# Attention with weight splitting: loads reordered, four weight chunks per slot, one threshold comparison moved to VectorE

## What is computed

```python
scores = scale * q @ k.T
kth = the 32nd largest of each row
scores = where(scores >= kth, scores, -1e9)
attn = exp(scores - max) / (sum + 1e-9)
x = (attn @ v), heads side by side           # 2304 x 512
out = ((x @ w_a) * (x @ w_b)) @ w_out
```

## Time and profile before

| | us |
|---|---|
| median of 3 runs | 920.54 (920.47 to 922.51) |
| the profiled execution | 920.49 |
| its span in the trace | 918.6 |
| TensorE matmul busy | 832.0 (91%) |
| VectorE busy | 725.4 (79%) |
| ScalarE busy | 593.5 (65%) |
| GpSimd busy | 736.1 (80%) |

### The profile page before, as it was taken

The page is one execution under the profiler, slowest core; times in us unless marked ns, Lnnn a source line. Parts: engine busy times, 40 slices in busy tenths (PEclk is TensorE's granted clock), DMA queues, the critical chain, the costliest instruction groups (busy, mean ns, idle before and its releaser), DMA issues.

```text
span 918.6 us, 17902 instructions
## 1 busy us (share of the span) xinstructions
PE 832.0 (91%) x6368; PEld 682.5 (74%) x6368; DVE 725.4 (79%) x1595; ACT 593.5 (65%) x1296; POOL 736.1 (80%) x618
## 2 busy tenths in 40 slices
PE   2357668999999999999999999999999999999998
PEld 1134446887788888877888888877888888888897
DVE  2778889997798999977999898888988999995000
ACT  3466667666677776666766776666677777775322
POOL 3699998987788889877888888877888888889232
PEclk9999999999999999999999999999999999999999
DMA  6422431112331121122321211123222111211221
GB/s 167 127 72 75 143 111 52 41 43 67 80 90 41 53 59 47 44 66 73 96 54 41 65 41 42 48 60 102 67 55 64 50 47 42 61 35 47 70 60 56
DMA packets 83175, 60.92 MB, mean 66 GB/s; under 512 B 60816, under 2 KB 60816, under 8 KB 83088
## 3 DMA queue, kind: packets, MB, share of 16 engines
q1 hardware_dynamic: 83088, 59.79, 23.5%
HBM read 51.90 MB, written 7.86 MB: 65 GB/s over the span
## 4 chain that ended last, share of the span: by engine, by line
PE 71%; POOL 12%; ACT 7%; issue 5%; DVE 2%; DMA 1%; SPq 1%; ACTq 0%; POOLq 0%
PE ps L428 31%; PE ps L441 14%; PE ps L396 7%; PE ps L373 7%; PE ps L363 6%; POOL keep L641 5%; POOL scores L649 4%; POOL w_lo L628 2%; ACT scores L528 2%; PE ps L359 1%; ACT scores L521 1%; ACT probs_t L545 1%; PE ps L388 1%; ACT scores L536 1%; DMA stage<-in_w 1%
## 5 line engine op out<-in xcount | busy, mean ns | idle before, releaser
L641 POOL TENSOR_SCALAR keep<-scores,best 128x576 f32<-128x576 f32 x144 | 319.1, 2216 | 11.2 <-POOL scores L649 5.9
L707 DVE MAX8 best<-work 128x8 f32<-128x576 f32 x432 | 304.6, 746 | 0.0
L428 PE MATMUL ps<-x_hi,w_hi 128*128 128x256 f32 x864 | 262.9, 304 | 3.1 <-ACT x_lo L555 3.1
L428 PE MATMUL ps<-x_hi,w_lo 128*128 128x256 f32 x864 | 243.3, 282 | 0.0
L428 PE MATMUL ps<-x_lo,w_hi 128*128 128x256 f32 x864 | 243.0, 281 | 0.0
L717 DVE MATCH_REPLACE8 work<-best,work 128x576 f32<-128x576 f32 x288 | 211.6, 742 | 0.0
L649 POOL TENSOR_TENSOR scores<-scores,keep 128x576 f32<-128x576 f32 x144 | 204.4, 1419 | 3.5
L428 PEld LDWEIGHTS ps<-x_hi,w_hi 128*128 128x128 f32 x864 | 162.5, 188 | 35.4 <-issue 26.9
L428 PEld LDWEIGHTS ps<-x_lo,w_hi 128*128 128x128 f32 x864 | 163.1, 189 | 0.9
L428 PEld LDWEIGHTS ps<-x_hi,w_lo 128*128 128x128 f32 x864 | 162.6, 188 | 0.0
L655 POOL TENSOR_TENSOR ab<-ab 128x256 f32<-128x256 f32 x108 | 79.4, 735 | 84.3 <-ACT ab L561 84.3
(11 more groups left out here) (50 smaller groups left out, 1050.8 us busy)
## 6 DMA issues: line engine op xcount, KB each, us to landing
wo_lo<-x_scratch SPq DMA_DIRECT2D x108, 256.0 KB, 2.7
stage<-in_w SPq DMA_DIRECT2D x36, 256.0 KB, 2.8
q_rows<-in_q SPq DMA_DIRECT2D x72, 64.0 KB, 2.6
k_rows<-in_k SPq DMA_DIRECT2D x32, 128.0 KB, 2.4
v_rows<-in_v SPq DMA_DIRECT2D x32, 128.0 KB, 2.5
out<-stage SPq DMA_DIRECT2D x15, 256.0 KB, 2.6
x_scratch<-wo_lo SPq DMA_DIRECT2D x12, 256.0 KB, 2.0
out<-stage SPq DMA_DIRECT2D x6, 128.0 KB, 2.4
```

Source lines behind the costliest of these rows:

```text
L428: last = mm(ps_ab[:, which, :], w[:, c, o:o + P], x[:, g % 2, kb, :], start=(kb == 0 and i == 0), stop=(kb == KB - 1 and i == 2))
L641: V.tensor_scalar(keep[:], scores[:, u % ROWS, j, 0:S], best[:, u % 2, j, TOPK - 1:TOPK], NEG, ALU.is_lt, ALU.mult).then_inc(keep_ready, 1)
L707: ins = V.max(best[:, s % 2, j, 8 * r:8 * r + 8], src)
```

## The change

Three things are done, for the slots up to 8 only.

- Loads: SyncE starts with K of both first pairs, then Q of unit 1, then four weight chunks; each pair of V is loaded in a slot of its own, -2 to 1. Q of unit 0 is issued by ScalarE, ahead of its first instruction.
- Weights: four chunks in each of slots 0 to 8 and none before slot 0, with four `stage` buffers instead of three. So `between(s, 0)` now holds a chunk too.
- Comparison: for units 0 to 7, VectorE compares tile 0 (L733 of the changed kernel) behind the search of its unit, into `work`, tile 0, which that search no longer needs; GpSimd adds it to the scores right behind `shifts`, ahead of the slot's first cut. VectorE's first replacement in tile 0 of the next unit, which writes `work`, waits for that mask (`mask_done`). Tile 1 stays on GpSimd.

```diff
--- before.py
+++ after.py
@@ -34,7 +34,6 @@
     WB0 = KB * DFF // WC
     WO0 = 2 * WB0
     ROWS = 4
-    STAGES = 3
     RING = 4
     QBUF = 3
 
@@ -71,7 +70,7 @@
                 at += 1
             PREP_AT[at] = (b, p)
     PREPS = [PREP_AT[at] for at in sorted(PREP_AT)]
-    V_AT = {}
+    V_AT = {p - 2: [(0, p)] for p in range(KB)}
     for b in range(1, BATCHES):
         for p in range(KB):
             V_AT.setdefault(last_unit(b - 1, p) + 3, []).append((b, p))
@@ -97,12 +96,10 @@
     def o_step(F):
         return 3 * (F + 2) + 2
 
-    W_COUNT = {-2: 3, -1: 4, 0: 5, 1: 3, 2: 3, 3: 3, 4: 3, 5: 3, 6: 3, 7: 3, 8: 3}
-    W_AT, w_next = {}, 0
-    for s in sorted(W_COUNT):
-        W_AT[s] = list(range(w_next, w_next + W_COUNT[s]))
-        w_next += W_COUNT[s]
-    assert w_next == WCH
+
+    W_EACH = 4
+    STAGES = 4
+    W_AT = {s: list(range(s * W_EACH, (s + 1) * W_EACH)) for s in range(WCH // W_EACH)}
 
     def w_of(s, n, parts):
         mine = W_AT.get(s, [])
@@ -123,6 +120,7 @@
         w_lo = sb("w_lo", [P, WO0, WC], fp32r)
         wo_lo = sb("wo_lo", [P, RING, WC], fp32r)
         stage = sb("stage", [P, STAGES, WC])
+        y = stage
         ident = sb("ident", [P, P])
         neg_ident = sb("neg_ident", [P, P], fp32r)
         k_rows = sb("k_rows", [P, NB, P])
@@ -145,7 +143,6 @@
         ab = sb("ab", [P, 2, 2, G])
         h_hi = sb("h_hi", [P, 2, G], fp32r)
         h_lo = sb("h_lo", [P, 2, G], fp32r)
-        y = stage
 
         ps = ctx.enter_context(nc.psum_tensor("ps", [P, 8, 512], fp32))
         ps_s = ps[:, 0:2, 0:HALF]
@@ -176,6 +173,7 @@
         chain = sem("chain")
         kth_ready = sem("kth_ready")
         keep_ready = sem("keep_ready")
+        early_ready = sem("early_ready")
         mask_done = sem("mask_done")
         e_ready = sem("e_ready")
         inv_ready = sem("inv_ready")
@@ -204,10 +202,15 @@
         def is_tail(u):
             return UNITS[u][1] == FULL
 
+
+        def compared_early(u, j):
+            return j == 0 and u + 1 in W_AT
+
         def preps_before(u):
             b, t, pairs, place = UNITS[u]
             return max(PREPS.index((b, p)) for p in pairs) + 1
 
+        EARLY = [u for u in range(NU) if compared_early(u, 0)]
         PIECES = []
         for g in range(GROUPS):
             pieces = []
@@ -240,7 +243,7 @@
                              ).then_inc(ld_k, 16)
 
             def load_q(u):
-                if not unit(u):
+                if not unit(u) or u == 0:
                     return
                 b, t, pairs, place = UNITS[u]
                 wait(sp, qt_done, u - QBUF + 1)
@@ -297,13 +300,10 @@
                         store_y(F // NF)
 
             load_k(0)
-            load_q(0)
+            load_k(1)
+            load_q(1)
             for c in range(STAGES):
                 load_w(c)
-            load_q(1)
-            load_k(1)
-            for p in range(KB):
-                load_v(0, p)
             for s in range(FIRST, LAST):
                 for b, p in V_AT.get(s, []):
                     load_v(b, p)
@@ -589,6 +589,8 @@
                 for c in w_of(s, part, 4):
                     split_hi(c)
 
+            act.dma_start(q_rows[:, 0, 0:2 * D].rearrange("p (h d) -> p h d", h=2),
+                          q[0:2, 0:P, :].rearrange("h p d -> p h d")).then_inc(ld_q[0], 16)
             act.wait_ge(s_ident, 2)
             A.mul(neg_ident[:], ident[:], -1.0).then_inc(s_negid, 1)
             copy_k(0)
@@ -626,7 +628,6 @@
                     wait(pool, st_wo[n % RING], 16 * (n // RING))
                     to = wo_lo[:, n % RING, :]
                 V.tensor_tensor(to, stage[:, c % STAGES, :], w_hi[:, c, :], ALU.subtract).then_inc(w_lo_done, 1)
-
             def shifts(u):
                 if not unit(u):
                     return
@@ -634,7 +635,7 @@
                 V.tensor_scalar(neg_max[:, u % 2, :], best[:, u % 2, :, 0], -SCALE, None, ALU.mult)
 
             def below(u, j):
-                if not unit(u):
+                if not unit(u) or compared_early(u, j):
                     return
                 pool.wait_ge(kth_ready, 2 * u + j + 1)
                 wait(pool, mask_done, 2 * u + j)
@@ -645,7 +646,11 @@
                 if not unit(u):
                     return
                 row = scores[:, u % ROWS, j, 0:S]
-                pool.wait_ge(keep_ready, 2 * u + j + 1)
+                if compared_early(u, j):
+                    pool.wait_ge(early_ready, EARLY.index(u) + 1)
+                    V.tensor_tensor(row, row, work[:, j, :], ALU.add).then_inc(mask_done, 1)
+                    return
+                pool.wait_ge(keep_ready, sum(not compared_early(n // 2, n % 2) for n in range(2 * u + j + 1)))
                 V.tensor_tensor(row, row, keep[:], ALU.add).then_inc(mask_done, 1)
 
             def after_step(n):
@@ -672,9 +677,12 @@
                             pattern=[[-1, P]], channel_multiplier=1).then_inc(s_ident, 1)
             for s in range(FIRST, LAST):
                 shifts(s - 1)
+                if unit(s - 1) and compared_early(s - 1, 0):
+                    masked(s - 1, 0)
                 below(s - 1, 0)
                 between(s, 0)
-                masked(s - 1, 0)
+                if unit(s - 1) and not compared_early(s - 1, 0):
+                    masked(s - 1, 0)
                 between(s, 1)
                 below(s - 1, 1)
                 between(s, 2)
@@ -714,10 +722,16 @@
                         for j in range(2 if r < ROUNDS - 1 else 0):
                             src = scores[:, s % ROWS, j, 0:S] if r == 0 else work[:, j, :]
                             dve.wait_ge(chain, found[j])
+                            if r == 0 and unit(s - 1) and compared_early(s - 1, j):
+                                dve.wait_ge(mask_done, 2 * (s - 1) + j + 1)
                             V.match_replace(out=work[:, j, :], in_to_replace=best[:, s % 2, j, 8 * r:8 * r + 8],
                                             in_values=src, imm_value=NEG).then_inc(chain, 1)
                             count += 1
                             replaced[j] = count
+                    if compared_early(s, 0):
+                        dve.wait_ge(kth_ready, 2 * s + 1)
+                        V.tensor_scalar(work[:, 0, :], scores[:, s % ROWS, 0, 0:S], best[:, s % 2, 0, TOPK - 1:TOPK], NEG,
+                                        ALU.is_lt, ALU.mult).then_inc(early_ready, 1)
                 if unit(s - 1):
                     wait(dve, e_ready, 2 * (s - 1) + 2)
                     V.tensor_scalar(sums_eps[:], sums[:, (s - 1) % 2, :], EPS, None, ALU.add).then_inc(chain, 1)
```

## The result

| | us |
|---|---|
| before, median of 4 runs | 921.52 (920.47 to 922.52) |
| changed kernel, median of 4 runs | 906.63 (906.11 to 907.09) |
| ratio | 0.9838, 95% interval 0.9821 to 0.9855 |
| the profiled execution of the changed kernel | 907.07, span 905.3 |

The change is 14.9 us faster. The forecast was 905.8 us, with a range of 901.5 to 909.8.

A forecast was written before the change was run, and what follows sets the result against it. A chain through VectorE, ScalarE and GpSimd bounds early slots, TensorE the rest. Start at 33.0 plus seven slots 84.09 plus 2.4 gives 119.5 against 134.21, 14.7 earlier: 920.49 - 14.7 = 905.8 us, range 901.5 to 909.8.

The forecast's parts named there:

- The ring: Early slots: VectorE's reciprocal, ScalarE's casts, GpSimd's cuts and mask, then back; 10.55 plus 1.45 us set the 12.0 us slot.
- the hole: GpSimd's 0.61 us idle ahead of its cut at 79.21 in the kernel before, waiting for ScalarE's cast.
- That cover: ScalarE's 0.66 us wait for TensorE hides the new 0.62 us cast; without it, 0.6 us more a slot.
- The comparison at a bad place: VectorE's comparison runs behind GpSimd's mask of tile 1 and delays the slot's last cut: 0.4 us in six slots, 2.4 us.
- D(n): Start of VectorE's addition to the sums, which ends unit n; forecast 33.0 us for unit 0, 119.5 for unit 7.
- let in only when GpSimd idles: Rival, chance 0.10: VectorE's comparison comes after GpSimd's cut and shift, costing 0.95 us a slot, 5.7 in six; 909.8 us.
- VectorE's price: The moved comparison's own time on VectorE, shown by no row: taken as 0.4 us, between 0.169 and 0.746.
- The start: Loads in order of need, no weights ahead of unit 0: first addition to the sums 17.1 us earlier, at 33.0.
- the 0.7 us to spare: Slack of GpSimd's side at the start: exponential at 32.3 us, ahead of the first addition to the sums at 33.0.
- the start gains less: Rival, chance 0.14: weights of slot 1 land 3 us late, first addition to the sums at 35.3; 908.1 us.
- The block behind slot 9: Slots from the tenth on, paced by TensorE, stay unchanged and move whole, 14.7 us earlier; 775 us from the first product.
- The shortened slots: Rival, chance 0.07: GpSimd's own work is the bound, so slots fall to VectorE's 10.64 us; 893.8 us.

The follow-up runs named there:

- masks first: The changed kernel with GpSimd's order turned in slots 0 to 8, both masks ahead of all four cuts: 897.75 us, against 906.63 for the change.

## Why the prediction was right

- *The ring.* Shown. Period, place of the hole and the part that each engine has agree within 0.13 us: from the reciprocal's end, 70.97, to the mask's end, 81.65, 10.68 us against 10.55. The new cast went into ScalarE's wait for TensorE: from the normalisation to the next cast 3.76 us, before 3.77. That cover was measured in hundredths, and it held.
- *The comparison at a bad place.* The mechanism was right and its size too large: 0.23 us a slot where I put 0.4. What made the slot 12.37, near my 12.4, is the open 0.12 us. The count was off too: D(n) is the start of the addition, and the wait lies inside it (0.54 us at 33.10, 0.31 at 119.67), so the wait at D(0) already lengthens the first of the seven slots. It is seven times 0.35 us, 2.48 in the trace, where I put six times 0.4, 2.4: that the sum came out is luck. Between VectorE held and GpSimd held, the rows of before showed one half; the stretched cut shows the other. The rule of the Trainium skill ("SBUF — State Buffer", "SBUF: two separate sides"), that the pair of ports is locked for the whole instruction and the other blocks fully, agrees with both. The rival that it is let in only when GpSimd idles is out: it ended 0.32 us behind the mask, with a cut waiting.
- *VectorE's price.* 0.51 us undisturbed, for 0.4 assumed, within the bounds of 0.17 and 0.75. The Trainium skill ("VectorE: DVE Perf Modes", on the TRN2 errata) gives 58 cycles and half a cycle an element at 0.96 GHz, an estimate of 0.36 us for 576 elements, and adds that the 58 come out short against a measured fixed term of about 150 cycles, by which the estimate is 0.46 us. The trace is above both.
- *The start.* D(0) was forecast at 33.0 and came at 33.10, by luck, through two errors of opposite sign. VectorE started 0.6 us earlier (Q was there at 9.47, not 10.0). But not VectorE's side decided, as I had it: ScalarE's first cast of slot 1 waited for its load until 24.06.

```profile
24.06 0.62 ACT L488 CAST w_hi<-stage 128x512 fp32r<-128x512 f32 x1 [1.92 <-DMA stage<-in_w]
```

The cut behind it came at 24.75 instead of 24.05, which used up the 0.7 us to spare, and VectorE stood idle for 0.61 us ahead of D(0). The rival "the start gains less" was this near.
- *The block behind slot 9.* Here a step failed: "the rest moves as a block". From D(7) on it moved 1.24 us less in the profiled execution (14.54 us at D(7), 13.3 us in the span), since TensorE went through slot 9 at its lower level and lost 1.69 us up to the first product; 0.45 us came back behind it. I had read one profile with the clock full in all slices and not asked how fast its products ran, slot by slot, nor whether that would come out the same again. Between the two profiled executions the gain is therefore 13.4 us (920.49 to 907.07). That the medians give 14.9, so near my 14.7, has luck in it: I had started from 920.49, the low end of the runs of before, whose median beside the change was 921.52.
- *The rivals.* The shortened slots (893.8 us) need another order than this change has: masks first took 9 of those 12 us.

## What to carry to other kernels

An engine that is busy 11 of 12 us may still not be what sets the 12: look for its waits, follow the one releaser back until the chain closes, and only work on that chain counts. Work taken off such an engine buys little until the chain is cut, and the cut may be a mere change of order (9 us here, with nothing removed). Where an engine's new instruction shares something with a neighbour, ask at which moment of the neighbour's it arrives.

## What the runs showed of the hardware

- A tensor-scalar instruction of VectorE waits for the end of GpSimd's instruction under way, and GpSimd's next one waits in turn: 0.51 us alone, 0.97 to 1.25 in the change, 1.47 where it met a cut of 1.26 at its start, each time ending 0.32 us behind the end of GpSimd's instruction in the slots shown; the cut behind it 1.49 instead of 1.27.
- The same comparison over 128 x 576 takes 2.22 us on GpSimd and 0.51 on VectorE.
- TensorE's pace ahead of the second stage differs from slot to slot and from kernel to kernel, and the mean granted clock of one kernel from run to run (0.957 to 1.000): 20 products with V take 2.40 us in one slot and 1.31 us in the next, in slot 9 of the change 2.40 and in that of the kernel before 1.31. In these stretches the granted clock reads 0.50 in the change and 1.00 in the profile of before. What makes the two profiles differ stays open. The 1.00 of the profile of before doesn't show the lower level: its slot 8 has products of 2.40 us under it.
